# An expert stage cut into 47 blocks of 256 tokens and 9 blocks of 128, instead of 55 blocks of 256

## The reference

```
X = fft(fft(x, axis=1), axis=2).real                       # stage A
xn, en = x / (|x| + 1e-6), emb / (|emb| + 1e-6)             # stage B, 8 experts
logits = xn @ en.T / tau; e = argmax(logits); g = softmax(logits)[e]
out[token] = g * (relu(x @ w1[e]) @ w2[e])                  # w1 256 x 1024, w2 1024 x 256
xk, xr = mixes of x and the previous token                  # stage C
out = sigmoid(xr @ w_r) * (relu(xk @ w_k)**2 @ w_v)
```

## Time and profile before

| | |
|---|---|
| profiled execution | 1442.9 us, of which the span from first to last instruction is 1440.9 us |
| TensorE busy | 1403.9 us, 97% of the span |
| weight loads busy | 1282.2 us, 89% |
| VectorE / ScalarE / GpSimd busy | 1088.1 (76%) / 872.3 (61%) / 250.8 us (17%) |
| DMA | 201.49 MB, mean 140 GB/s |
| mean granted clock of TensorE | 0.989 of full speed |
| expert stage | its first matmul starts 191.03 us into the span, its last group ends at 833.5 us |

### The profile page before, as it was taken

One profiled execution on the slowest core, in us unless ns is written; L12 is line 12 of the kernel. 1 busy time (PEld: TensorE's weight loads), 2 busy tenths in 40 slices (PEclk: granted clock), 3 DMA queues, 4 the chain that ended last, 5 costly groups with the idle time before them and its releaser, 6 DMA issues.

```text
span 1440.9 us, 27303 instructions
## 1 busy us (share of the span) xinstructions
PE 1403.9 (97%) x9048; PEld 1282.2 (89%) x9048; DVE 1088.1 (76%) x1815; ACT 872.3 (61%) x1687; POOL 250.8 (17%) x225
## 2 busy tenths in 40 slices
PE   8999989998999999999999969999999999999998
PEld 7988879998999999999999958888888888888886
DVE  4788887876776777777677657878788887878784
ACT  2665576665766666666666546656565666656563
POOL 2154537551331111111111100000000000000000
PEclk8999999999999999999999989999999999999999
DMA  8334378899667677777766322212131313131201
GB/s 243 84 102 130 119 240 277 270 292 322 221 212 226 218 219 218 228 240 235 227 216 219 132 45 40 49 32 55 29 58 29 58 29 58 29 58 29 57 17 29
DMA packets 208343, 201.49 MB, mean 140 GB/s; under 512 B 189641, under 2 KB 191543, under 8 KB 199672
## 3 DMA queue, kind: packets, MB, share of 16 engines
q1 hardware_dynamic: 197336, 175.18, 42.9%
q0 software_dynamic: 9888, 25.28, 5.3%
q10 hardware_dynamic: 1056, 0.26, 0.1%
HBM read 160.44 MB, written 42.06 MB: 141 GB/s over the span
## 4 chain that ended last, share of the span: by engine, by line
PE 91%; DVE 3%; DMA 2%; SPq 1%; ACT 1%; issue 1%; POOL 0%; ACTq 0%; POOLq 0%; DVEq 0%
PE ps L626 82%; PE ps L654 3%; PE ps L694 3%; PE ps L679 1%; DMA we_raw<-w_e 1%; PE ps L680 1%; DMA rows<-xr,pos 1%; DVE zu L1171 1%; DVE zv L1171 1%; SPq L455 0%; DVE we L1146 0%; SPq L540 0%; DMA xm<-moe 0%; ACT we L817 0%; PE ps L631 0%
## 5 line engine op out<-in xcount | busy, mean ns | idle before, releaser
L626 PE MATMUL ps<-x_split,w_split 128*128 128x512 f32 x1440 | 332.3, 391 | 11.3 <-DVE x_split L1293 11.3
L626 PE MATMUL ps<-we,ht 128*128 128x256 f32 x2640 | 328.7, 283 | 4.8 <-DVE ht L1229 4.8
L626 PEld LDWEIGHTS ps<-x_split,w_split 128*128 128x128 f32 x1440 | 271.6, 189 | 68.1 <-issue 11.5
L626 PE MATMUL ps<-xgt,we 128*128 128x256 f32 x2640 | 324.7, 282 | 4.3 <-DVE we L1146 4.3
L626 PEld LDWEIGHTS ps<-we,ht 128*128 128x128 f32 x2640 | 322.1, 189 | 6.4 <-DVE ht L1229 6.1
L626 PEld LDWEIGHTS ps<-xgt,we 128*128 128x128 f32 x2640 | 319.4, 190 | 4.7 <-issue 4.7
L1146 DVE TENSOR_TENSOR we<-we_raw,we 128x1024 fp32r<-128x1024 f32 x220 | 263.9, 1221 | 22.6 <-ACT we L817 22.1
L626 PE MATMUL ps<-k_split,w_split 128*128 128x512 f32 x1152 | 265.0, 389 | 0.0
L626 PEld LDWEIGHTS ps<-k_split,w_split 128*128 128x128 f32 x1152 | 216.2, 188 | 44.9
L1229 DVE SCALAR_TENSOR_TENSOR ht<-ps,ht 128x512 fp32r<-128x512 f32 x220 | 146.1, 684 | 144.4 <-ACT ht L878 144.2
L817 ACT CAST we<-we_raw 128x1024 fp32r<-128x1024 f32 x220 | 225.1, 1048 | 8.3 <-DMA we_raw<-w_e 8.3
(11 more groups left out here) (131 smaller groups left out, 1085.4 us busy)
## 6 DMA issues: line engine op xcount, KB each, us to landing
we_raw<-w_e SPq DMA_DIRECT2D x55, 2048.0 KB, 8.3
xg<-rows SPq DMA_DIRECT2D x220, 64.0 KB
out<-yc SPq DMA_DIRECT2D x96, 128.0 KB, 2.7
xm<-moe SPq DMA_DIRECT2D x94, 128.0 KB, 2.8
xin<-x SPq DMA_DIRECT2D x15, 768.0 KB, 6.5
rows<-tailc SPq DMA_DIRECT2D x9, 258.0 KB, 9.2
moe<-yo,meta POOLq DMA_INDIRECT x110
rows<-xr,pos POOLq DMA_INDIRECT x96, 2.7
```

The source lines that it names most:

```text
L626: ins = mm(o, a(i), b_(k), start=first_ and n == 0, stop=last_ and n == 2)
```

## The change

Blocks come in two sizes. NP = 47 blocks ("pairs") have 256 tokens and NS = 9 ("ones") have 128, 56 blocks in all. The ones are blocks 21, 25, 29, ... 53: after the 18 blocks written out, the loop has nine turns of four blocks (MIX = 4), three pairs and a one; two more pairs follow. Each expert's rows are first cut into whole 256s, what remains is rounded up to 128s; an odd unit of 128 becomes a one, and ones that no expert needs get halves of spare pairs.

- **A one** (`tokens(i)` = 128): the matmuls of `up` have 128 moving columns instead of 256, still 48 of them; its chunks are still four, each half as wide; `down` makes one tile, 24 matmuls. Hidden values, rows, results and the scatter are halved. Its weights (2 MB to load and to split) are whole.
- **Lists**: `tier_a(True)` and `tier_a2` run behind block 4, `tier_b` and `tier_c` behind block 5, `tier_d` and `tier_e` behind block 6, and five new pieces behind blocks 7 to 11, which find the ones' experts and rows. The last of them, `tier_spare2` behind block 11, ends with the third increment of `d_tier`.
- **Tails**: `load_tails` stands where it stood and waits for `d_tier` 3 instead of 2.
- Waits count by `at_`, `ahead`, `turn` and `scattered_ahead`, which give the same counts for mixed sizes.

```diff
+NS = 9
+NP = (B * S // P + E - 1 - NS) // 2
+NB = NP + NS
+MIX = 4
+TIERS = ((0, 17), (17, NP - 17))
...
+        def one(i):
+            return i[1] == MIX - 1 if isinstance(i, tuple) else LEAD <= i < LEAD + MIX * NS and (i - LEAD) % MIX == MIX - 1
+        def tokens(i):
+            return P if one(i) else BT
...
+        def blocks(eng, step):
+            for i in range(LEAD):
                 step(i, i % 2)
+            with eng.Fori(0, NS) as t:
+                for r in range(MIX):
+                    step((t, r), r % 2)
+            for i in range(LEAD + MIX * NS, NB):
                 step(i, i % 2)
...
             def load_meta(i, s):
...
                 if i >= LEAD + 2:
-                    sp.wait_ge(scattered[s], i // 2 * (16 * HB))
+                    sp.wait_ge(scattered[s], scattered_ahead(i, s))
...
             def load_tails():
-                sp.wait_ge(d_tier, 2)
+                sp.wait_ge(d_tier, 3)
...
             def up(i, s):
...
-                        last = mm3(ps[:, f // 2, (f % 2) * BT:(f % 2 + 1) * BT],
+                        last = mm3(ps[:, f // 2, (f % 2) * n:(f % 2 + 1) * n],
                                    lambda a: w1_[a][:, c, f * P:(f + 1) * P],
-                                   lambda k: xgt[:, k, c, :], c == 0, c == DC - 1)
+                                   lambda k: xgt[:, k, c, 0:n], c == 0, c == DC - 1)
...
             def down(i, s):
...
-                for j in range(HB):
+                for j in range(n // P):
...
-                for j in range(HB):
+                for j in range(tokens(i) // P):
                     result(i, s, j)
...
                     if i == 4:
                         tier_a(True)
+                        tier_a2(True)
                     if i == 5:
-                        tier_a2(True)
+                        tier_b(True)
+                        tier_c(True)
                     if i == 6:
-                        tier_b(True)
+                        tier_d(True)
+                        tier_e(True)
                     if i == 7:
-                        tier_c(True)
+                        tier_odd()
                     if i == 8:
-                        tier_d(True)
+                        tier_odd2()
                     if i == 9:
-                        tier_e(True)
+                        tier_odd3()
+                    if i == 10:
+                        tier_spare()
+                    if i == 11:
+                        tier_spare2()
...
+            def tier_spare2():
+                total_odd = sums[1][:, 4 + E:5 + E]
+                t_link(v.tensor_scalar(late1[:], iota[0:1, 0:NS], total_odd, None, ALU.is_ge))
+                for out_, h, none, dst in ((where1, 0, E * CAPR, row_of), (who1, 1, E - 1, expert_of)):
+                    t_link(v.scalar_tensor_tensor(out_[:], late1[:], -float(none), out_[:], ALU.mult, ALU.add))
+                    t_link(v.tensor_tensor(out_[:], out_[:], got1[:, h, :], ALU.add))
+                    end = copy(dst[:, mixed].rearrange("o (t r) -> o t r", r=MIX)[:, :, MIX - 1], out_[:])
+                end.then_inc(d_tier, 1)
```

More of the change, by code:

```diff
@@ L425, in d_bank, with at_, after, ahead @@
             return 2 * ((c + 1) % 3)
-        def pairs(eng, lead, n, step):
-            for i in range(lead):
-                step(i, i % 2)
[L431 to L435, removed]
+        def one(i):
+            return i[1] == MIX - 1 if isinstance(i, tuple) else LEAD <= i < LEAD + MIX * NS and (i - LEAD) % MIX == MIX - 1
+        def tokens(i):
+            return P if one(i) else BT
+        def at_(i):
+            return i[0] * MIX + (LEAD + i[1]) if isinstance(i, tuple) else i
+        def after(i):
+            return (i[0], i[1] + 1) if isinstance(i, tuple) else i + 1
+        def ahead(i, of_pair, of_one):
+            if isinstance(i, tuple):
+                t, r = i
+                return t * ((MIX - 1) * of_pair + of_one) + ((LEAD + min(r, MIX - 1)) * of_pair + r // MIX * of_one)
+            ones = sum(one(k) for k in range(i))
+            return (i - ones) * of_pair + ones * of_one
+        def turn(i):
+            return i[0] * (MIX // 2) + (LEAD // 2 + i[1] // 2) if isinstance(i, tuple) else i // 2
+        def scattered_ahead(i, s):
+            if isinstance(i, tuple):
+                t, r = i
+                return t * (16 * (4 if s == 0 else 3)) + 16 * HB * (LEAD // 2 + r // 2)
+            return sum(16 * (1 if one(k) else HB) for k in range(s, i, 2))
+        def blocks(eng, step):
+            for i in range(LEAD):
+                step(i, i % 2)
+            with eng.Fori(0, NS) as t:
+                for r in range(MIX):
+                    step((t, r), r % 2)
+            for i in range(LEAD + MIX * NS, NB):
                 step(i, i % 2)
@@ L544, in _ @@
             for n in range(2):
-                sp.wait_ge(scattered[n], 16 * HB * len(range(n, NB, 2)))
+                sp.wait_ge(scattered[n], scattered_ahead(NB + (NB - n) % 2, n))
             out_flat = out.rearrange("b s d -> (b s) d")
@@ L742, in m_step @@
                 down(i, s)
-            pairs(pe, LEAD, NB, m_step)
+            blocks(pe, m_step)
             for n in range(2):
                 pe.wait_ge(s_split[n], len(C_SPLIT_AT))
-            pe.wait_ge(m_y, NB * HB)
+            pe.wait_ge(m_y, ahead(NB, HB, 1))
             def c_step(t, s):
@@ L823, in rows_a @@
             def rows_a(i):
[L824 to L825 removed]
+                act.wait_ge(m_xf, at_(i) + 1)
+                copy(xgt[:, 0, :, 0:tokens(i)], xgf[:, :, 0:tokens(i)]).then_inc(m_xh, 1)
             def squares(b, k2):
@@ L891, in m_step @@
                 more = not isinstance(i, int) or i + 1 < NB
-                hidden_a(i, 0)
+                for n in range(FC // 2):
+                    hidden_a(i, n)
+                    if more and n < 2:
+                        w_high_part(after(i), 1 - s, n)
                 if more:
[L894 to L903, removed]
+                    rows_a(after(i))
+                    w_high_part(after(i), 1 - s, 2)
+                    w_high_part(after(i), 1 - s, 3)
                 if isinstance(i, int) and i in C_SPLIT_AT:
@@ L915, in m_step @@
                     exponential(B - 1)
-                for j in range(HB):
+                for j in range(tokens(i) // P):
                     result(i, s, j)
-            pairs(act, LEAD, NB, m_step)
+            blocks(act, m_step)
             for n in range(2):
-                act.wait_ge(scattered[n], 16 * HB * len(range(n, NB, 2)))
+                act.wait_ge(scattered[n], scattered_ahead(NB + (NB - n) % 2, n))
             for n in range(2):
@@ L1086, in tier_a2, with running @@
                     t_link(copy(tail_at[:], run[:]))
-            def tier_b(last):
-                t_link(copy(sums[0][:, 5:5 + E], avail[:]))
+            def running(n):
+                t_link(copy(sums[0][:, 5:5 + E], n))
                 a, z = sums
@@ L1094, in tier_b @@
                     a, z = z, a
+                return a
+            def tier_b(last):
+                running(avail[:])
             def tier_take():
@@ L1235, in m_step @@
                 if more:
-                    rows_t(i + 1, 1 - s)
-                hidden_v(i, 0)
-                if more:
[L1239 to L1248, removed]
+                    rows_t(after(i), 1 - s)
+                for n in range(FC // 2):
+                    hidden_v(i, n)
+                    if more and n < 2:
+                        w_low_part(after(i), 1 - s, n)
+                if more:
+                    rows_v(after(i), 1 - s)
+                    w_low_part(after(i), 1 - s, 2)
+                    w_low_part(after(i), 1 - s, 3)
                 if isinstance(i, int):
@@ L1376, in scatter @@
             def scatter(i, s):
-                pool.wait_ge(meta_in[s], 16 * (i // 2 + 1))
-                for j in range(HB):
-                    pool.wait_ge(m_y, i * HB + (j + 1))
+                pool.wait_ge(meta_in[s], 16 * (turn(i) + 1))
+                for j in range(tokens(i) // P):
+                    pool.wait_ge(m_y, ahead(i, HB, 1) + (j + 1))
                     g.indirect_dma_start(out=moe_flat, in_=yo[s][:, j, :], in_offset=None,
```

157 lines of the change are left out of this document (106 added, 51 removed).

## The result

The changed kernel takes 1470.79 us, the median of four runs (1469.25 to 1473.42), against 1440.62 us for the kernel before beside it. The ratio is 1.0211, with a 95% interval of 1.0192 to 1.023. It is 30 us slower; 1467 us was forecast. The profiled execution has a span of 1467.5 us, 26.6 more than before.

A forecast was written before the change was run, and what follows sets the result against it. TensorE, busy 97% of the span, was taken to bound the kernel. Late weights +6 us and tail wait +20 us gave +26 on 1442.9 us, so 1467 us for the median; range 1446 to 1500.

The forecast's parts named there:

- The matmuls: Expert stage on TensorE: eight pairs go, nine ones of 8.14 us come, at 0.110 us a narrow matmul; alone -18.3 us.
- The rival of slow narrow matmuls: `up` of the ones: 0.230 us a matmul, 13.9 us a one, stage +33.4 us, 1494 us in all; chance 0.20.
- The late weights: Loop: weights of the block after next land 3.0 us late, one and next pair take 22.3 us; stage +6 us.
- The term of +6 us: Expert stage: 38 pairs at 11.45 us and nine one-and-pair couples at 22.3 us give 635.8 against 629.9 us.
- I take no clock loss: Pairs behind ones: stalls are two pieces of 1.3 us or less, so no clock loss was counted in the +6 us.
- The bound of +19.5: Upper bound of the late-weights term: 6 + 9 x 1.5 us, if the clock falls at each of these stalls.
- the rival with a loss in each of the nine: Loop: as forecast, but each late load also drops the clock, +13.5 us, 1480 us; chance 0.09.
- The tails wait: Blocks 12 and 13: first tail issues 23.2 us later, delaying block 13's weights behind it in SyncE's queue; +20 us.
- The lower bound of 15: Tail wait at blocks 12 and 13: 15 us if tails issue and land faster with no weights in flight beside them.
- The lists: VectorE behind blocks 4 to 11: up to 2.4 us of small instructions a block, cost on the path 0.

The follow-up runs named there:

- 3: Changed kernel, but from block 19 on SyncE issues the weights of block i+2 ahead of the meta load of block i+1: 1439.39 us, ratio 0.998.
- 5: Kernel before, without small blocks, with the weights issued ahead of the meta load from block 19 on: 1441.06 us, ratio 0.9991.
- 1: Changed kernel, but the tails wait for the second list and only block 15 waits for the third: 1457.61 us, ratio 1.0107.
- 2: Kernel before, without small blocks, with the last piece of its second list behind block 11 instead of 9: 1455.73 us, ratio 1.0082.
- 4: Changed kernel with tails waiting for the second list and, from block 19, weights issued ahead of the meta load: 1423.91 us, ratio 0.9868.

## Why the prediction was right

- **The matmuls.** 0.110 us a narrow matmul was forecast from stage A, 0.111 measured; 8.14 us a one, 8.22 to 8.24 in eight of nine. The rival of slow narrow matmuls (0.230) is out: the type that had no row of this width goes at the pace of its weight load, 0.112 us in this trace (48 loads in 5.45 us). The estimate of 107 ns by the Trainium skill (TensorE: Matmul & The Clock Gate, LDWEIGHTS) is near; its 81 ns a pair (the same page, Back-to-back issue gap) is not reached.
- **The late weights.** Forecast: there 13.3 us into the one, one and pair 22.3 us. Measured: 13.3 on average (12.7 to 13.6, and 15.1 in the first), and 22.2 on average in the five couples whose clock stays up. Runs 3 and 5 show the mechanism from both sides: the queue's order costs 33 us with small blocks and nothing that can be told without. That is more than the +11.7 below, because it also takes the 17.6 us that the small blocks save when their weights are in time: 29.3 of the 29.9 us between the two traces.
- **The clock, mis-sized.** The term of +6 us was measured at +11.7. "I take no clock loss" was the step that failed: four of the nine pairs ran at a mean granted clock of 0.89 and took 15.5 us on average, the other five 13.9. By their last matmuls, 36 took 5.9 us instead of 4.4 in three of them and 42 took 6.9 instead of 5.0 in the first: 6.3 us together, against an excess of 5.7. The forecast had reasoned from one short wait in block 12 that left the clock at 1.00, and that one case did not hold for these. The bound of +19.5 held it, and the rival with a loss in each of the nine, +13.5, was twice too dear.
- **The tails wait.** Forecast +20 us, measured +15.7. The chain is the forecast one: first tail at 334.63 (335.6 forecast), block 13's weights at 347.79 (351.4), landed at 355.5 (360.6), block 13 started at 366.22 (371.1), block 14 at 378.21 (383.3). Block 12 itself started 1.0 us earlier than before, at 333.50, so 1.0 us of each of these differences is not the wait's. The term too large was the length of the queue: first tail to weights took 13.2 us instead of 15.8 and the landing 7.7 instead of 9.2. That the tails had no weights in flight beside them fits (DMA engines busy 0.64 of the time while they went out, 0.97 before); for the landing it is not shown. The lower bound of 15 had named it. Runs 1 and 2 put the wait by itself at 15 and 14 us of time.
- **The lists** cost nothing on the path, as forecast: blocks 1 to 11 take what they took.
- The two errors, +5.7 and -4.3, nearly cancel, which is luck: 1467 us against 1470.79 is closer than its terms.

## What to carry to other kernels

Cutting a tile's compute cuts the time only if what the tile needs whole (here 2 MB of weights and their split) still arrives: before making a block shorter, work out from issue and landing how early its successor's load is, and what the load stands behind in its queue. A queue in program order makes every wait in it a wait for all that follows; put the load that is wanted next ahead of a wait that it does not need, and let a wait ask for no more than its operands. Such slack doesn't show in the old kernel's waits, since 0.35 us early and 5 us early look alike there.

## What the runs showed of the hardware

With idle stretches of TensorE of 0.76 to 2.58 us inside one block, its granted clock fell to 1.2 GHz in four pairs of nine (0.50 of full speed from 525.69 to 527.69, for one), in run 1 again in four of nine, and in none of nine when the stretches were partly filled; in the other pairs such stretches left it at 2.4 GHz. The length doesn't sort them: 0.94 and 0.76 us (pair at 514.44) went with a fall, 1.73 and 0.76 us (pair at 560.67) with none.

The tails land much sooner when they go out alone, by the page of the changed kernel (KB each, median us to landing):

```profile
rows<-tailc SPq DMA_DIRECT2D x9, 258.0 KB, 2.3
```

Before, when they went out right behind the weights of block 12, the same line had 9.2. The runs sort the same way: 2.4 and 2.5 in runs 2 and 3, where the tails went out alone, 9.1 and 9.0 in runs 1 and 4, where they did not.

A matmul with 128 columns of the split type goes every 0.111 us, one with 256 every 0.119: with the weights changed each time, half the columns save 7%.
